# An expert's second quarter of low weight parts, made ahead of the loads of its second half

## The chip, the cores and the metric

The kernel runs on one core of a Trainium2 chip. The metric is the time of one execution on the device in microseconds (us), the median of several runs.

## The reference

The program chains three stages. Its inputs and outputs are fp32.

```python
def _attn_ref(q, k, v, tau):            # 4 x 8 heads, 576 rows, 64 wide
    scores = scale * np.matmul(q, k.transpose(0, 1, 3, 2))
    thresh = np.max(scores, axis=-1, keepdims=True) - tau
    scores = np.where(scores >= thresh, scores, -1000000000.0)
    ...                                 # softmax, then attn @ v

def _moe_ref(x, expert_emb, tau, w1, w2):   # 2304 tokens x 512, 8 experts, F = 1024
    expert_idx = np.argmax(logits, axis=1)
    gate_w = probs[np.arange(N), expert_idx]
    for e in range(E):
        mask = expert_idx == e
        h = np.maximum(x[mask] @ w1[e], 0.0)
        out[mask] = gate_w[mask, None] * (h @ w2[e])

def _moe2_ref(x, w_in, w_out):          # 512 -> 2048 -> 512
    h = x @ w_in
    sp = np.where(h > 20.0, h, np.log1p(np.exp(np.minimum(h, 20.0))))
    return ((h * np.tanh(sp)) @ w_out).astype(np.float32)
```

The change is in the middle stage. With the given inputs the reference sends 213, 375, 233, 231, 281, 362, 418 and 191 tokens to experts 0 to 7.

## The kernel before

**Tokens and slots.** The router sorts the tokens by expert into slots of 128 rows; an expert gets as many slots as its tokens need, rounded up. From the counts above these are 2, 3, 2, 2, 3, 3, 4 and 2 slots, so that experts 0 to 7 begin at slots 0, 2, 5, 7, 9, 12, 15 and 19. The program always runs 25 slots (`SLOTS`); the four left over are worked with the last expert's weights. `start_i` holds the first slot of each expert, `sexp_i` the expert of each slot.

**TensorE** walks the slots in order (`slot(i)` in the TensorE block): `m1` of slot i (x @ w1 in 8 groups), the transposes `t_x` of slot i+1's tokens (L1106), `m2` of slot i-1 (h @ w2), and the transposes `t_h` of slot i's hidden values (L1136). Each product is three fp32r matmuls (`passes`, L1110 to L1112): high part of the data times high part of the weights, high times low, low times high. So for each weight the kernel needs a high part `wh` and a low part `wl`.

**Weights.** An expert has 4 MB of them, handled in 16 chunks of 128x512 (`CH_E`), four chunks to a quarter (`CQ`). Quarters 0 and 1 are w1, quarters 2 and 3 are w2. Each weight is read twice:

- The *high part* comes by a cast load from HBM, fp32 to fp32r, one DMA of 1 MB for each quarter, issued by POOL (`load_quarter`, L605). It goes into one of two halves of `wh`, by the parity of the expert.
- The *raw values* come by DMAs of 256 KB from SP's queue (`chunk`, L475) into `stage`, a ring of four chunks. SP may issue chunk n when POOL has used chunk n-4 (it waits on `w_split`).
- The *low part* is then made by POOL: stage minus wh, one TENSOR_TENSOR for each chunk (`low_parts`, L594, called through `low_quarter`), which counts up `w_split`. It waits for the cast load of its quarter and for its chunk in `stage`.

**What TensorE waits for.** `m1` of a slot of expert e waits for `w_split` to reach 16 e + 8 (quarters 0 and 1 of that expert's low parts are made); `m2` waits for 16 e + 12, and from its fifth group on for 16 e + 16.

**POOL's order.** Experts 0 and 1 are mostly handled during attention and routing. From expert 2 on, POOL runs `next_expert(e, par, n)` once for each expert, in program order: for e = 2 and 3 written out, for 4 to 7 in a hardware loop with two experts in its body. Its steps are

1. wait until `m1` of expert e-2 is done (`m1_done`), then issue the cast loads of quarters 0 and 1 of expert e (here called point A);
2. make the low parts of quarter 3 of expert e-1, then of quarter 0 of expert e;
3. wait until `m2` of expert e-2 is done (`m2_done`), then issue the cast loads of quarters 2 and 3 of expert e (point B);
4. make the low parts of quarters 1 and 2 of expert e.

In the first two of these, POOL also issues the gathers of token rows that are not yet in (`gather`, L631): two after point A of expert 2, five behind expert 2's last low part. POOL, SP and the DMA queues keep the order in which the program names them.

Of the kernel before, what the change touches and what calls it, by code (L numbers as in the profile page):

```python
# [82 lines left out]
def build(nc, qT, kT, v, tau, embT, moe_tau, w1, w2, w_in, w_out, out):  # L83
# [446 lines left out]
    def _(g):  # L530
# [52 lines left out]
        def low_parts(use, high, low, first, chunks=range(CH_E)):  # L583


            for c in chunks:
                if c % CQ == 0 and first[c // CQ] is not None:
                    g.wait_ge(*first[c // CQ])
                g.wait_ge(stg_in[c % STAGES], (use + c // STAGES + 1) * 16)
                src, dst = high(c), low(c)  # L590
                raw = stage[:, c % STAGES, :]
                if len(src.shape) == 3:
                    raw = raw.rearrange("p (a b) -> p a b", a=src.shape[1])
                g.tensor_tensor(dst, raw, src.bitcast(F32), ALU.subtract).then_inc(w_split, 1)  # L594

        def load_quarter(e, par, i):
            a = i * CQ * CHUNK
            dst = wh[:, par, a:a + CQ * CHUNK]
            if i < 2:
                src = w1_e[e, :, 2 * i:2 * i + 2, :]  # L600
                dst = dst.rearrange("p (k f) -> p k f", k=KD // 2)
            else:
                src = w2_e[e, :, (i - 2) * CQ:(i - 1) * CQ, :]
                dst = dst.rearrange("p (c n) -> p c n", c=CQ)
            g.dma_start(dst, src).then_inc(w_cast[par][i], 16)  # L605
# [8 lines left out]
        def low_quarter(e, par, n, i):  # L614

            low_parts(CH_E // STAGES * e,
                      lambda c: wh[:, par, c * CHUNK:(c + 1) * CHUNK],
                      lambda c: wl[:, 1 - par, c * CHUNK:(c + 1) * CHUNK],
                      [(w_cast[par][j], 16 * n) for j in range(QUARTERS)], range(i * CQ, (i + 1) * CQ))
# [9 lines left out]
        def gather(s):  # L629
            got = x_first[s] if s < FIRST else x_near if s < NEAR else x_far if s < FAR else x_next if s < AHEAD else x_last  # L630
            g.indirect_dma_start(x_slot(s), None, x_tok, bass.IndirectOffsetOnAxis(inv_i[:, s:s + 1], 0),  # L631
                                 bounds_check=N - 1, oob_is_err=False).then_inc(got, 16)
# [11 lines left out]
        def next_expert(e, par, n):  # L644

            first = g.value_load(start_i[0:1, bass.ds(e - 1, 1)], min_val=1, max_val=SLOTS)
            g.wait_ge(m1_done, g.snap(first * 2))
            g.sem_inc(pool_passed, 1)
            load_quarter(e, par, 0)
            load_quarter(e, par, 1)  # L650
            if isinstance(e, int) and e == 2:
                for s in range(FAR, AHEAD):
                    gather(s)
            low_quarter(e - 1, 1 - par, n - 1 + par, 3)
            low_quarter(e, par, n, 0)
            g.wait_ge(m2_done, first)
            g.sem_inc(pool_passed, 1)
            load_quarter(e, par, 2)
            load_quarter(e, par, 3)
            low_quarter(e, par, n, 1)  # L660
            low_quarter(e, par, n, 2)

        next_expert(2, 0, 2)
        for s in range(AHEAD, SLOTS):
            gather(s)
        next_expert(3, 1, 2)
        with g.Fori(2, E // 2) as b:
            for par in range(2):
                next_expert(b * 2 + par, par, b + 1)
# [950 lines left out]
```

## Time and profile before

| | |
|---|---|
| median of 3 runs | 1066.23 us (1063.78 to 1070.02) |
| profiled execution, its own time | 1065.5 us |
| its span, first to last instruction | 1063.9 us |
| mean granted TensorE clock | 0.987 of full speed |
| TensorE busy, of the span | 1023.2 us, 96% |
| POOL busy, of the span | 587.7 us, 55% |
| busy in low parts of the experts (L594, `wl`) | 162.8 us, 128 chunks |
| idle of POOL before these | 56.0 us, of which 50.1 us until a chunk had landed in `stage` |
| TensorE idle until a low part was made | 3.4 us, once |

A row of a list of groups reads: line, engine, operation, output<-inputs, shapes, count, busy time and mean ns of one, then the idle time of that engine just before them and what ended it. A busy share is an average over stages with different limits, so it does not tell by itself what an engine's work is worth: attention fills the first 300 us, the experts run from about 326 to 656 us, the last stage follows.

### The profile page before, as it was taken

The page shows a single profiled execution, that of the slowest core. Times are in us where ns is not written, and L with a number is a line of the kernel's source. Part 1 is how long each engine was busy: PE and PEld are TensorE (multiplying, and loading weights), DVE is VectorE, ACT ScalarE, POOL GpSimd, SP SyncE. Part 2 cuts the span into 40 slices and gives each one's busy share as a digit, 9 for nine tenths or more (in the row PEclk, how much of TensorE's full clock was granted, in tenths as well). Part 3 has the DMA queues.
Part 4 walks back from the last instruction along what each step waited for, and adds up shares of the span by engine and source line. Part 5 has one row for each costly group of instructions (what it writes and reads, how often), then busy time and mean ns, then how long its engine had stood idle before and what let it go on. Part 6 is the DMA issues. An engine that isn't in the chain of part 4 may idle for free.

```text
span 1063.9 us, 20987 instructions
## 1 busy us (share of the span) xinstructions
PE 1023.2 (96%) x6712; PEld 850.1 (80%) x6712; DVE 625.7 (59%) x1484; ACT 505.5 (48%) x1020; POOL 587.7 (55%) x672
## 2 busy tenths in 40 slices
PE   7999999999966999899999999999999999999996
PEld 5777777777634888788888889999999999999995
DVE  6998989898764222122222226776676676666653
ACT  5777777777653222222222224555545545555442
POOL 3344444444345868677660627776556565565564
PEclk9999999999987999999999999999999999999999
DMA  8165425441065899998871736400000100000000
GB/s 200 40 169 161 120 81 152 127 125 44 12 220 149 247 287 279 293 295 266 291 240 47 264 104 208 119 31 21 27 14 31 31 10 20 30 30 0 9 22 31
DMA packets 97526, 128.87 MB, mean 121 GB/s; under 512 B 34400, under 2 KB 51808, under 8 KB 96928
## 3 DMA queue, kind: packets, MB, share of 16 engines
q1 hardware_dynamic: 72544, 66.54, 21.8%
q0 software_dynamic: 18880, 53.22, 15.8%
q10 hardware_dynamic: 6016, 7.96, 2.1%
q8 instruction: 53, 0.87, 0.3%
q14 instruction: 33, 0.27, 0.1%
HBM read 111.70 MB, written 16.00 MB: 120 GB/s over the span
## 4 chain that ended last, share of the span: by engine, by line
PE 59%; POOL 4%; DMA 4%; issue 2%; DVE 2%; ACT 1%; another core or an unknown queue 0%; POOLq 0%; SPq 0%; ACTq 0%; DVEq 0%
PE ps L1110 18%; PE ps L1111 18%; PE ps L1112 18%; DMA stage<-w 4%; POOL wl L594 3%; PE ps L1136 1%; PE ps L1048 1%; POOL wh L605 1%; PE ps L1185 1%; PE ps L1106 1%; POOL xs_far L631 1%; PE ps L1058 1%; ACT junk L824 1%; PE ps L997 0%
## 5 line engine op out<-in xcount | busy, mean ns | idle before, releaser
L594 POOL TENSOR_TENSOR wl<-stage,wh 128x512 fp32r<-128x512 f32 x128 | 162.8, 1294 | 56.0 <-DMA stage<-w 50.1
L708 POOL TENSOR_TENSOR mg<-mw,mr 128x384 f32<-128x384 f32 x96 | 117.3, 1222 | 73.7 <-DVE mr L1545 73.2
L766 ACT ACTIVATE ex<-sc,rmin 128x576 f32<-128x576 f32 x144 | 111.6, 776 | 78.0 <-DVE sc L1316 78.0
L714 POOL TENSOR_TENSOR gl<-mg,gh 128x384 fp32r<-128x384 f32 x96 | 98.6, 1028 | 79.1 <-ACT gh L902 78.2
L1110 PE MATMUL ps<-yth,winh 128*128 128x384 f32 x384 | 130.9, 341 | 0.0
L1112 PE MATMUL ps<-yth,winl 128*128 128x384 f32 x384 | 129.5, 337 | 0.0
L1111 PE MATMUL ps<-ytl,winh 128*128 128x384 f32 x384 | 128.8, 335 | 0.0
L1326 DVE SCALAR_TENSOR_TENSOR pm<-sc,thr,ex 128x576 f32<-128x576 f32 x144 | 116.7, 812 | 19.2 <-POOL thr L558 15.3
L1316 DVE TENSOR_SCALAR_CACHE_REDUCE sc<-ps,nscale 128x576 f32<-128x576 f32 x144 | 116.9, 813 | 9.8 <-PE ps L957 9.0
L558 POOL TENSOR_SCALAR thr<-rmin,taup 128x1 f32<-128x1 f32 x144 | 75.4, 524 | 76.2 <-DVE sc L1316 74.2
L1111 PE MATMUL ps<-woutl,gh 128*128 128x512 f32 x288 | 113.5, 394 | 0.0
L1110 PE MATMUL ps<-wouth,gh 128*128 128x512 f32 x288 | 113.0, 392 | 0.0
L1112 PE MATMUL ps<-wouth,gl 128*128 128x512 f32 x288 | 111.9, 389 | 0.0
L894 ACT ACTIVATE ml<-mn,two 128x384 f32<-128x384 f32 x96 | 59.3, 617 | 97.7 <-DVE mn L1526 97.7
L1522 DVE TENSOR_SCALAR mm<-ps 128x384 f32<-128x384 f32 x96 | 53.3, 555 | 88.2 <-PE ps L1112 88.1
L1483 DVE TENSOR_TENSOR xtl<-ps,xth 128x512 fp32r<-128x512 f32 x25 | 17.3, 692 | 130.5 <-ACT xth L839 118.7
L1005 PE MATMUL ps<-pt,vb 128*64 128x128 f32 (+1 forms) x1280 | 93.4, 282 | 0.0
L890 ACT ACTIVATE mm<-mm 128x384 f32<-128x384 f32 x96 | 50.3, 524 | 90.0 <-DVE mm L1522 89.8
L1110 PE MATMUL ps<-wh,xth 128*128 x200 | 81.8, 409 | 7.5 <-POOL wl L594 3.4
L957 PE MATMUL ps<-k_t,q_t 64*128 64x288 f32 x512 | 81.7, 439 | 5.9 <-DMA k_t<-kT 5.9
L854 ACT ACTIVATE hth<-ps 128x512 fp32r<-128x512 f32 x50 | 27.2, 596 | 126.4 <-PE ps L1136 121.1
L1005 PEld LDWEIGHTS ps<-pt,vb 128*64 128x64 f32 (+1 forms) x1280 | 67.0, 135 | 21.6 <-issue 21.6
(193 smaller groups left out, 2253.0 us busy)
## 6 DMA issues: line engine op xcount, KB each, us to landing
stage<-w SPq DMA_DIRECT2D x128, 256.0 KB, 4.5
wh<-w POOLq DMA_DIRECT2D x32, 1024.0 KB, 8.1
y_dense<-yo ACTq DMA_DIRECT2D x25, 256.5 KB
q_t<-qT SPq DMA_DIRECT2D x16, 288.0 KB, 3.6
k_t<-kT SPq DMA_DIRECT2D x16, 288.0 KB, 4.1
vb<-v SPq DMA_DIRECT2D x16, 288.0 KB, 4.5
stage<-w_in SPq DMA_DIRECT2D x16, 256.0 KB, 3.4
winh<-w_in POOLq DMA_DIRECT2D x1, 4096.0 KB, 13.8
```

The source lines that it names most:

```text
L558: g.tensor_scalar(thr[:, i % 2, t:t + 1], rmin[:, i % 2, t:t + 1], taup[:, :], None, ALU.add).then_inc(thr_ready, 1)
L594: g.tensor_tensor(dst, raw, src.bitcast(F32), ALU.subtract).then_inc(w_split, 1)
L708: g.tensor_tensor(mg[:, f % 2, :], mw[:, f % 2, :], mr[:, f % 2, :], ALU.mult).then_inc(g_done, 1)
L714: g.tensor_tensor(gl[:, f % 4, :], mg[:, f % 2, :], gh[:, f % 4, :].bitcast(F32), ALU.subtract).then_inc(gl_ready, 1)
L766: act.activation(ex[:, i % 2, t * S:(t + 1) * S], sc[:, i % 2, t * S:(t + 1) * S], ACT.Exp, bias=rmin[:, i % 2, t:t + 1], scale=-1.0).then ...
L957: m = pe.matmul(s_psum(lane)[:, h, :], q_t[st // HEADS][rows, st % HEADS, q0:q0 + P], k_t[rows, st, h * S // 2:(h + 1) * S // 2], start=Tr ...
L1005: m = pe.matmul(ps[to, OT0:OT0 + P], vb[rows, st, k, :], pt[rows, i % 2, k * P:(k + 1) * P], start=c == 0, stop=c == PAIRS)
L1110: pe.matmul(out_, lhs_h, rhs_h, start=start, stop=False)
L1111: pe.matmul(out_, lhs_h, rhs_l, start=False, stop=False)
L1112: return pe.matmul(out_, lhs_l, rhs_h, start=False, stop=stop)
L1316: dve.tensor_scalar(sc[:, i % 2, t * S:(t + 1) * S].rearrange("p (h n) -> p h n", h=2), s_psum(t), nscale[:, :], BIG, ALU.mult, ALU.min, a ...
L1326: dve.scalar_tensor_tensor(pm[:, i % 2, t * S:(t + 1) * S], sc[:, i % 2, t * S:(t + 1) * S], thr[:, i % 2, t:t + 1], ex[:, i % 2, t * S:(t ...
```

## The change

In `next_expert` the call that makes quarter 1 of the low parts moves from behind point B to ahead of the wait for `m2_done` that stands before it.

```diff
@@ def next_expert(e, par, n):
             low_quarter(e - 1, 1 - par, n - 1 + par, 3)
             low_quarter(e, par, n, 0)
+            low_quarter(e, par, n, 1)
             g.wait_ge(m2_done, first)
             g.sem_inc(pool_passed, 1)
             load_quarter(e, par, 2)
             load_quarter(e, par, 3)
-            low_quarter(e, par, n, 1)
             low_quarter(e, par, n, 2)
```

The order of the chunks, their number and their buffers stay. On all engines but POOL the instructions are the same in the same order. On POOL, for experts 2 and 3, the program before has these instructions (x8 under one row are two quarters of low parts; L605 with 128x2x1024 is a cast load of a w1 quarter, with 128x4x512 of a w2 quarter):

```order
L605 DMA wh<-w 128x2x1024 x2
L631 DMA xs_far<-x_tok,inv_i 128x512 x2
L594 TENSOR_TENSOR wl<-stage,wh 128x512 x8
L605 DMA wh<-w 128x4x512 x2
L594 TENSOR_TENSOR wl<-stage,wh 128x512 x8
L631 DMA xs_far<-x_tok,inv_i 128x512 x5
...
L605 DMA wh<-w 128x2x1024 x2
L594 TENSOR_TENSOR wl<-stage,wh 128x512 x8
L605 DMA wh<-w 128x4x512 x2
L594 TENSOR_TENSOR wl<-stage,wh 128x512 x8
```

In the changed program twelve low parts stand between the two pairs of loads, and four between the second pair and the next expert's first. The same place, with the change:

```order
L605 DMA wh<-w 128x2x1024 x2
L631 DMA xs_far<-x_tok,inv_i 128x512 x2
L594 TENSOR_TENSOR wl<-stage,wh 128x512 x12
L605 DMA wh<-w 128x4x512 x2
L594 TENSOR_TENSOR wl<-stage,wh 128x512 x4
L631 DMA xs_far<-x_tok,inv_i 128x512 x5
...
L605 DMA wh<-w 128x2x1024 x2
L594 TENSOR_TENSOR wl<-stage,wh 128x512 x12
L605 DMA wh<-w 128x4x512 x2
L594 TENSOR_TENSOR wl<-stage,wh 128x512 x4
```

The loads of the w2 quarters moved behind one quarter more of low parts; the loads of the w1 quarters kept their place.

In the loop body, which stands for experts 4 to 7, the same quarter moved past the same pair of loads (one of the two copies; ISA rows are waits with a register's value):

```order
 L594 TENSOR_TENSOR wl<-stage,wh 128x512 x4
+L589 ISA
+L594 TENSOR_TENSOR wl<-stage,wh 128x512 x4
 L605 DMA wh<-w 128x4x512 x2
-L589 ISA
-L594 TENSOR_TENSOR wl<-stage,wh 128x512 x4
 L589 ISA
 L594 TENSOR_TENSOR wl<-stage,wh 128x512 x4
```

## Rows read from the trace of the kernel before

**Rows 1.** The page: two engines' busy time, and the group of low parts.
```profile
PE 1023.2 (96%) x6712; PEld 850.1 (80%) x6712; DVE 625.7 (59%) x1484; ACT 505.5 (48%) x1020; POOL 587.7 (55%) x672
L594 POOL TENSOR_TENSOR wl<-stage,wh 128x512 fp32r<-128x512 f32 x128 | 162.8, 1294 | 56.0 <-DMA stage<-w 50.1
```

**Rows 2.** Who TensorE waited for, 380 to 800 us: total, times, longest.
```profile
PE ps L1110 <- POOL wl L594: 3.4, 1, 3.4
```

**Rows 3.** The chain that ended last, 402 to 446 us: start, us, what.
```profile
405.50 1.51 POOL wh L605 x2
407.03 3.80 POOL wl L594 x3
410.85 7.02 DMA stage<-w
...
437.02 1.51 POOL wh L605 x2
438.55 4.96 POOL wl L594 x4
443.70 0.49 PE ps L1110
```

**Rows 4.** POOL in order of time, 361 to 453 us: start, us, what, [idle before].
```profile
361.80 5.05 POOL L594 TENSOR_TENSOR wl<-stage,wh 128x512 fp32r<-128x512 f32 x4 [3.08 <-DMA stage<-w]
366.78 1.59 POOL L605 DMA_DIRECT2D wh<-w  x2
...
376.85 2.68 POOL L594 TENSOR_TENSOR wl<-stage,wh 128x512 fp32r<-128x512 f32 x2 [3.28 <-DMA stage<-w]
379.84 2.55 POOL L594 TENSOR_TENSOR wl<-stage,wh 128x512 fp32r<-128x512 f32 x2 [0.32 <-DMA stage<-w]
...
405.50 1.51 POOL L605 DMA_DIRECT2D wh<-w  x2
...
415.16 5.32 POOL L594 TENSOR_TENSOR wl<-stage,wh 128x512 fp32r<-128x512 f32 x4 [2.56 <-DMA stage<-w]
420.42 1.42 POOL L605 DMA_DIRECT2D wh<-w  x2
...
437.02 1.51 POOL L605 DMA_DIRECT2D wh<-w  x2
438.55 4.95 POOL L594 TENSOR_TENSOR wl<-stage,wh 128x512 fp32r<-128x512 f32 x4
447.37 5.04 POOL L594 TENSOR_TENSOR wl<-stage,wh 128x512 fp32r<-128x512 f32 x4 [3.86 <-DMA stage<-w]
452.33 1.42 POOL L605 DMA_DIRECT2D wh<-w  x2
```

**Rows 5.** TensorE in order of time: slots 7, 9, 10 and 12 begin.
```profile
415.41 0.48 PE L1110 MATMUL ps<-wh,xth 128*128 x1
...
439.29 1.04 PE L1136 MATMUL ps<-ident,hs 128*128 128x128 f32 x8
443.70 0.49 PE L1110 MATMUL ps<-wh,xth 128*128 x1 [3.37 <-POOL wl L594]
...
457.71 0.48 PE L1110 MATMUL ps<-wh,xth 128*128 x1
...
482.38 0.48 PE L1110 MATMUL ps<-wh,xth 128*128 x1
```

**Rows 6.** Stretches of 4 us: engines' busy us (x), PEclk, DMA share, GB/s.
```profile
436.00:440.00 4.00, 4.00 (x23) 3.33 (x22) 0.32 (x2) 0.08 (x1) 3.98 (x5) 1.00 0.75 199
444.00:448.00 4.00, 4.00 (x12) 3.20 (x12) 0.00 (x0) 0.00 (x0) 0.63 (x1) 0.61 1.13 377
```

**Rows 7.** DMA issues of stretches at 437, 532, 432 and 440: last number, us to landing.
```profile
wh<-w POOLq DMA_DIRECT2D x1, 1024.0 KB, 7.2
wh<-w POOLq DMA_DIRECT2D x1, 1024.0 KB, 9.0
stage<-w SPq DMA_DIRECT2D x1, 256.0 KB, 3.6
stage<-w SPq DMA_DIRECT2D x1, 256.0 KB, 7.4
```

**Rows 8.** Same view at 175 us and at 636 us; then POOL in order of time there.
```profile
wh<-w POOLq DMA_DIRECT2D x1, 1024.0 KB, 5.3
wouth<-w_out POOLq DMA_DIRECT2D x1, 1024.0 KB, 5.7
636.44 1.50 POOL L695 DMA_DIRECT2D wouth<-w_out  x2 [11.88 <-PE ps L1112]
642.25 7.95 POOL L594 TENSOR_TENSOR woutl<-stage,wouth 128x512 fp32r<-128x512 f32 x6 [4.31 <-DMA wouth<-w_out]
```

## The prediction

> **What bounds the kernel now.** I read the page first: TensorE is busy for 96% of the span, POOL for 55% [rows 1]. So a change on POOL can only pay where TensorE waits for POOL. The list of TensorE's waits shows one such place behind 380 us: 3.4 us, once, for a low part of the weights [rows 2]. The chain of waits shows what stands ahead of it: until 443.70 it runs along POOL and the loads into `stage`, from there on along TensorE [rows 3]. TensorE in order of time names the place: it ends slot 8 with the transposes that start at 439.29 and last 1.04 us, and starts the next m1 at 443.70 [rows 5]. That is slot 9, the first of expert 4, whose m1 needs quarters 0 and 1 of that expert's low parts; POOL ends quarter 1 at 438.55 + 4.95 = 443.50 [rows 4]. The need arises at 439.29 + 1.04 = 440.33.
>
> The stall has a second cost. Between 444 and 448 the granted clock is 0.61, against 1.00 before it [rows 6], so part of that stretch ran at the lower of the two levels (1.2 GHz) after TensorE had stood idle. Slot 9 lasts 457.71 - 443.70 = 14.01 us, where slots 10 and 11 take (482.38 - 457.71) / 2 = 12.33 each [rows 5]: 1.7 us lost. So whatever brings expert 4's quarter 1 forward wins at most 3.4 + 1.7 = 5.1 us (0.5%), and whatever delays it costs its delay in full, since nothing later gives it back. I count half a per cent, 5.3 us, as what a measurement of this kernel can tell from no change.
>
> **What sets POOL's pace.** Call A the issue of an expert's first two cast loads, B that of the second two. B stands at 366.78, 405.50 and 437.02 for experts 2, 3 and 4, A at 420.42 and 452.33 for experts 4 and 5 [rows 4]: B to A takes 14.9 and 15.3 us, A to B 16.6. Of the low parts POOL is idle 56 us, 50.1 of it for chunks in `stage` [rows 1]. The first low part of quarter 2 starts late behind B: 376.85 - 366.78 = 10.1, 415.16 - 405.50 = 9.7, 447.37 - 437.02 = 10.4 us [rows 4]. These 10 us hold the two issues (1.5), quarter 1 (5.0) and some 3 us of waiting for chunk 8. That chunk was asked for when chunk 4 was used, and lands 7.4 us after its issue, against 3.6 for one issued at 432, when no cast load was under way [rows 7]. The cast load of quarter 2, issued at 437, has landed in 7.2 us by then [rows 7], hidden behind quarter 1.
>
> **The change, part by part.** Nothing is added or removed: the same 16 low parts, 4 cast loads and 16 chunks for each expert. Three things move.
>
> 1. Quarter 1 comes ahead of the two issues of B. It starts 1.5 us earlier against quarter 0's end, whose chunks are unaffected: they are loaded against A's casts as before. Its own chunks were asked for as quarter 0's were used, with no cast under way, at 3.6 us each; four low parts last 4 x 1.3 = 5.2 us [rows 1], so each chunk has 3.9 us. I take 5.2 us and no wait. The gain is 1.5 us, once, in front of each expert's m1.
>
> 2. B comes 5.2 us later. The wait for `m2_done` ahead of it was over at the earlier B of experts 2 to 4 already (POOL's rows show no idle time there [rows 4]), so it costs nothing 5 us later. SP's queue is not held by it.
>
> 3. Quarter 2 now has no cover: POOL issues B's pair and next needs what the first of them brings. The chunks are no longer the limit, since they were asked for during quarter 1. The trace does not show this order with `wh`, so I bound L, the time from B's first issue to quarter 2's first low part. From below: the fastest cast load of all landed in 5.3 us. The nearest row is w_out's at 636: a pair of 1 MB casts, rows of the same shape, POOL idle behind them, the first landed in 5.7, first low part 642.25 - 636.44 = 5.8 us after the issue [rows 8]. There, no chunk was under way; here the last two of quarter 2's are (issued 1.3 and 0 us before B), and at 377 GB/s [rows 6] 256 KB take 0.7 us. So I take L = 6.5. From above: a first-of-pair under load took 7.2, the slowest 9.0 [rows 7].
>
> The Trainium skill has a rule that speaks against this change: "DMA: Bandwidth & Descriptors", Rules for kernel authors, says to issue a DMA early, compute, and wait for it late. Rows 3 to 5 show the order before doing just that, and by this rule the time goes up.
>
> **The sum.** Before, B to quarter 2 took about 10.1; now quarter 0's end to quarter 2 takes 5.2 + L = 11.7. That is lost for every expert, and it adds up, as A and B follow POOL. With quarter 0 of expert 2 ending as before at 366.8:
> - expert 2: quarter 1 ends 372.0, quarter 2 starts 378.5 (376.85 before, +1.65); before, a 0.32 us wait stood in it [rows 4] that early chunks spare: +1.3. The five gathers and A of expert 3 move by that.
> - expert 3: quarter 0 ends 405.5 + 1.3 = 406.8, quarter 1 at 412.0, where slot 7 needs it at 415.41 [rows 5]: no stall. Quarter 2 starts 418.5 (415.16 before): +3.3.
> - expert 4: A 423.7, quarter 0 ends 437.0 + 3.3 = 440.3, quarter 1 at 445.5. Before: 443.5. So the stall grows from 3.4 to 5.4 us: **+2.0 us**.
>
> Behind it, each expert loses some 1.5 us more of POOL's lead. Expert 4's quarter 2 starts at 445.5 + 6.5 = 452.0 and ends at 457.2, A comes at 457.2 (452.33 before, +4.9). Expert 5's quarter 0 ended 15.7 us behind its A before, so now at 472.9, quarter 1 at 478.1; slot 12 needs it at 482.38 + 2.0 = 484.4. Six us are left, and experts 6 and 7, with more slots ahead of them, have more. The clock's loss of 1.7 us I keep. The profiled execution took 1065.5 us, so 1067.5; the median shown is 0.7 above it, so **1068.2**.
>
> **The rivals.**
>
> *Later still.* The pairs of casts now lie unevenly, B to the next A 12 us instead of 15, and meet chunks and stores of results; L becomes 7.2 to 9.0. With 7.2 the same walk gives delays of 2.0 and 4.8 us behind experts 2 and 3; expert 4's quarter 1 ends at 437.0 + 4.8 + 5.2 = 447.0, 3.5 us later than before: 1069.7. With 9.0 they are 3.8, 8.4, and 7.1 at expert 4: 1073.3. It passes 0.5% from L = 8.1 on. For it: two of three rows of loaded casts are near 8. Against it: the load that made those slow, the chunks of quarter 2, now comes first. 0.15.
>
> *Faster, the exposed cast is short.* If L is under 10.1 - 5.2 = 4.9 us, nothing is lost from expert to expert and the 1.5 us of the two issues remain as a gain: the stall is 1.9 us, 1064.7; if the clock then does not fall, 1.7 less, 1063.0. It decides at L = 4.9. Against it: no cast of 1 MB landed in under 5.3 us. 0.12.
>
> The same page (Anatomy of one DMA) gives 2.0 us plus bytes at 436 GB/s, 4.4 us as its estimate for 1 MB. By that L the time would be 1064.1, or 1062.4 with the clock kept. The rows disagree: 5.3 and 5.7.
>
> *Nothing.* L is 5.3 to 5.8 as on a quiet queue: -0.3 to +0.7 us at expert 4, 1066 to 1067. For it: the row at 636. 0.23, and 0.5 is left for my case with L from 5.8 to 7.2, 1066.9 to 1069.7.
>
> **How the numbers follow.** Likeliest 1068.2. The three runs of before lie from 1063.8 to 1070.0, so a median may be off by 1 to 2 us. The low end takes in half of the faster case, 1064.0; the high end most of the slow one, 1072.5. Faster by over 0.5% would be under 1060.9, beyond even the removal of the stall and its clock loss: 0.03. Slower by over 0.5% is over 1071.6, L above 8.1 with or without noise: 0.09. The rest, 0.88.
>
> **What would show it.** Right: on POOL twelve low parts without long waits in the last four; then two issues and an idle of 4 to 5.5 us before quarter 2, ended by the DMA `wh<-w` and no longer by `stage<-w`; A to A of 33 us instead of 31.9; TensorE's wait for `wl` of about 5.4 us at 440, once. Wrong: if that idle is under 3.4 us, or TensorE's wait is shorter than 3.4 or gone (faster case), if first-of-pair casts take over 7.2 us (later case), or if a second wait for `wl` appears at slot 7, 12 or 15, where I count 3 us or more in hand.

## The result, and the profile after

The changed kernel took 1073.02 us (median of 5 runs, 1069.68 to 1073.67) beside 1067.67 us before (5 runs, 1063.78 to 1070.02): ratio 1.0049, 95% interval 1.0029 to 1.0069. It is slower by 0.5%, 5.35 us between the medians, where 2.0 was forecast. Two more comparisons, among the experiments below, gave 1.0029 and 1.0045. The sign and the place were right, the size was not, and the median lies above the range's end of 1072.5. Of the 4.8 us between the forecast 1068.2 and the measured 1073.02, 3.4 are the size of the move; the other 1.4 are the level, for the median of before rose from 1066.23 to 1067.67 with its last two runs.

The profiled execution took 1069.68 us, its span 1068.0 us: 4.1 us more than the span before. It is the fastest of the five; the others took 1072.6 to 1073.7 us and left no trace. The page of the changed kernel, engines and low parts (before: [rows 1]):

```profile
PE 1024.9 (96%) x6712; PEld 851.3 (80%) x6712; DVE 626.5 (59%) x1484; ACT 505.2 (47%) x1020; POOL 585.6 (55%) x672
L594 POOL TENSOR_TENSOR wl<-stage,wh 128x512 fp32r<-128x512 f32 x128 | 161.9, 1292 | 68.5 <-DMA wh<-w 36.7
```

The work is the same: the same number of instructions on each engine, and busy times within 0.4% of those before. POOL's idle time ahead of low parts rose from 56.0 to 68.5 us, and its largest releaser changed: it was a chunk, `stage<-w`, now it is a cast load, `wh<-w`. TensorE's waits behind 380 us, where 3.4 stood [rows 2]:

```profile
PE ps L1110 <- POOL wl L594: 6.7, 1, 6.7
```

POOL in order of time in the changed kernel, experts 2 to 4, with the issues of the cast loads (L605) and the low parts (L594) (before: [rows 4]):

```profile
372.24 1.58 POOL L605 DMA_DIRECT2D wh<-w  x2
378.76 5.06 POOL L594 TENSOR_TENSOR wl<-stage,wh 128x512 fp32r<-128x512 f32 x4 [4.93 <-DMA wh<-w]
...
412.63 1.51 POOL L605 DMA_DIRECT2D wh<-w  x2
419.06 5.04 POOL L594 TENSOR_TENSOR wl<-stage,wh 128x512 fp32r<-128x512 f32 x4 [4.92 <-DMA wh<-w]
424.05 1.42 POOL L605 DMA_DIRECT2D wh<-w  x2
425.49 5.05 POOL L594 TENSOR_TENSOR wl<-stage,wh 128x512 fp32r<-128x512 f32 x4
435.18 8.70 POOL L594 TENSOR_TENSOR wl<-stage,wh 128x512 fp32r<-128x512 f32 x7 [4.65 <-DMA stage<-w]
445.29 1.26 POOL L594 TENSOR_TENSOR wl<-stage,wh 128x512 fp32r<-128x512 f32 x1 [1.41 <-DMA stage<-w]
446.49 1.51 POOL L605 DMA_DIRECT2D wh<-w  x2
```

Quarter 2 starts 378.76 - 372.24 = 6.5 and 419.06 - 412.63 = 6.4 us behind B, each time when the cast load has landed. B itself comes 5.5 and 7.1 us later than before. Quarter 1 of expert 4 ends at 445.29 + 1.26 = 446.55, 3.05 us later than the 443.50 of before, behind a chunk that was late by 1.41 us. TensorE in order of time, slots 9 and 10 (before: [rows 5]):

```profile
439.00 1.04 PE L1136 MATMUL ps<-ident,hs 128*128 128x128 f32 x8
446.74 0.79 PE L1110 MATMUL ps<-wh,xth 128*128 x1 [6.71 <-POOL wl L594]
...
461.66 0.48 PE L1110 MATMUL ps<-wh,xth 128*128 x1
```

Slot 9 lasts 461.66 - 446.74 = 14.92 us, where it lasted 14.01. The granted clock in stretches of 4 us (columns as in [rows 6]; the clock is the third number from the end) tells why:

```profile
444.00:448.00 4.00, 1.26 (x3) 1.14 (x4) 0.00 (x0) 0.00 (x0) 2.71 (x3) 0.50 0.67 178
448.00:452.00 4.00, 4.00 (x10) 3.06 (x10) 0.00 (x0) 0.00 (x0) 0.00 (x1) 0.50 1.06 312
452.00:456.00 4.00, 4.00 (x20) 3.33 (x19) 0.00 (x0) 1.48 (x3) 2.69 (x3) 0.96 0.96 279
```

TensorE idles from 440.0 on, and the clock stands at 0.50 (1.2 GHz) before the slot begins and until about 452, where before it was at full speed when slot 9 started and then fell for some 3 us (a mean of 0.61 over 444 to 448). So the later start (3.04 us) and the longer slot (0.91 us) make 3.95 of the 4.1 us.

### The profile page after: what moved, and what is told of

Read it like the earlier page. It is cut to its first block, busy times and chain, and to the rows that moved or that the text cites. A ratio compares the mean times of both kernels' runs of the same rounds, so it can differ in the third digit from the quotient of the medians.

```text
span 1068.0 us, 20987 instructions
## 1 busy us (share of the span) xinstructions
PE 1024.9 (96%) x6712; PEld 851.3 (80%) x6712; DVE 626.5 (59%) x1484; ACT 505.2 (47%) x1020; POOL 585.6 (55%) x672
## 4 chain that ended last, share of the span: by engine, by line
PE 64%; POOL 3%; issue 2%; DMA 2%; DVE 1%; ACT 1%; POOLq 0%; SPq 0%; ACTq 0%; DVEq 0%
PE ps L1110 20%; PE ps L1111 20%; PE ps L1112 20%; POOL wl L594 2%; PE ps L1136 2%; DMA stage<-w 2%; PE ps L1048 1%; PE ps L1106 1%; PE ps L1185 1%; PE ps L1058 1%; ACT junk L824 1%; POOL xs_far L631 0%; POOL wh L605 0%; PE ps L997 0%; POOLq L1588 0%
## 5 line engine op out<-in xcount | busy, mean ns | idle before, releaser
L594 POOL TENSOR_TENSOR wl<-stage,wh 128x512 fp32r<-128x512 f32 x128 | 161.9, 1292 | 68.5 <-DMA wh<-w 36.7
L846 ACT ACTIVATE hs<-ps 128x512 f32<-128x512 f32 x50 | 29.9, 598 | 116.3 <-PE ps L1112 116.3
```

## The experiments

My theory: the uncovered cast load of quarter 2 costs POOL time in experts 2 and 3, that time adds up until expert 4's m1, and the move itself gains 1.5 us there. All ratios are to the kernel before, on the same chip, with 95% intervals.

### The move for experts 4 to 7 only

In `next_expert`, e is a Python integer for experts 2 and 3, and a loop register for experts 4 to 7. Against the changed kernel:

```diff
+            early = not isinstance(e, int)
             low_quarter(e, par, n, 0)
-            low_quarter(e, par, n, 1)
+            if early:
+                low_quarter(e, par, n, 1)
             g.wait_ge(m2_done, first)
             ...
             load_quarter(e, par, 3)
+            if not early:
+                low_quarter(e, par, n, 1)
```

> The move is made only for experts 4 to 7; experts 2 and 3 keep the order before. My theory: the delay of the changed kernel is lost in experts 2 and 3 (exposed cast loads, +1.3 to +2 us each) and added up until expert 4's m1; the move itself brings expert 4's quarter 1 forward by 1.5 us. So TensorE's wait for wl at 440 falls from 3.4 to 1.9 to 2.6 us, and the time from the kernel before's by 0.8 to 1.5 us, up to 3.2 where the clock stays up (ratio 0.997 to 0.999). A to A of experts 5 to 7 still lengthens by 1.5 to 3 us without a wait of TensorE. Rival, the delay arises at expert 4 itself (its chunks or its loads): the wait is 5 us or more and the time is that of the changed kernel, ratio 1.003 to 1.006.

Measured: 1064.01 us, ratio 0.9976 (0.9959 to 0.9993), 2.3 us under the 1066.34 of before in the same comparison. That is faster than both kernels. TensorE's wait at slot 9 is 2.79 us, and POOL in order of time of this run shows quarter 0 and 1 of expert 4, then B and the exposed cast load behind them:

```profile
432.20 5.05 POOL L594 TENSOR_TENSOR wl<-stage,wh 128x512 fp32r<-128x512 f32 x4 [2.70 <-DMA stage<-w]
437.60 4.97 POOL L594 TENSOR_TENSOR wl<-stage,wh 128x512 fp32r<-128x512 f32 x4 [0.36 <-DMA stage<-w]
442.51 1.51 POOL L605 DMA_DIRECT2D wh<-w  x2
450.37 5.05 POOL L594 TENSOR_TENSOR wl<-stage,wh 128x512 fp32r<-128x512 f32 x4 [6.34 <-DMA wh<-w]
```

B to quarter 2 is 7.9 us here, and it costs nothing, for behind slot 9 TensorE does not wait for `wl` again. The wait is above the 1.9 to 2.6 expected: A of expert 4 stands at 423.02 here, 2.6 us later than in the first trace of before, behind waits of 1.9, 2.0 and 0.7 us for chunks in expert 3. The rival, a delay that arises at expert 4 itself, falls: the move is a gain there.

### The move for experts 2 and 3 only

The same edit, with the other experts chosen:

```diff
-            early = not isinstance(e, int)
+            early = isinstance(e, int)
```

> The move is made only for experts 2 and 3; experts 4 to 7 keep the order before. My theory: point A of expert 4 comes at about 424 us as in the changed kernel, its point B at 440.7, quarter 1 ends 6.5 us later, at 447.2 or more; TensorE's wait for wl is 7 to 8 us, longer than in the changed kernel (6.7), and the time 3.7 to 4.5 us plus some 1 us of clock over the kernel before, ratio 1.004 to 1.006. Rival, the delay arises at expert 4 itself: wait 3.4 us, ratio 1.000.

Measured: 1071.57 us, ratio 1.0052 (1.0036 to 1.0068), 5.2 us over before in the same comparison. The list of its waits:

```profile
PE ps L1114 <- POOL wl L594: 9.1, 1, 9.1
```

The wait is above the 7 to 8 us expected: L of expert 3 was 8.0 us, where the changed kernel's first trace has 6.4 (B at 413.19, quarter 2 at 421.22). The loss is made in experts 2 and 3 alone. The two halves of the move, +5.2 and -2.3 us, add up to 2.9 us, a little under the 3.2 to 5.35 us that the three comparisons of the whole change give.

### The pair of loads split

```diff
             g.wait_ge(m2_done, first)
             g.sem_inc(pool_passed, 1)
             load_quarter(e, par, 2)
+            low_quarter(e, par, n, 1)
             load_quarter(e, par, 3)
-            low_quarter(e, par, n, 1)
             low_quarter(e, par, n, 2)
```

> Point B is split: cast load of quarter 2, low parts of quarter 1, cast load of quarter 3, low parts of quarter 2. My theory: the loss of the change is the cast load of quarter 2 without cover; here quarter 1 covers it (5.2 us of 5.7) and the chunks of quarter 2 meet one cast load instead of two, so quarter 2 starts about 7 to 8 us behind B instead of 9.7 to 10.4. Expert 2 and 3 then gain some 2 us each, expert 4's quarter 1 ends before 441 and TensorE's wait is 0 to 1 us: time 3 to 5 us under the kernel before, ratio 0.995 to 0.997. Rival, the loads as a whole (8 MB an expert) set the pace of POOL: whatever quarter 2 wins the next quarters lose by later loads, A to A stays at 31 to 32 us, ratio 0.999 to 1.001.

Measured: 1061.67 us, ratio 0.9960 (0.9942 to 0.9978). One of the 12 executions took 3516.9 us, for a reason that no trace shows; the others lie between 1059.9 and 1066.9. POOL in order of time of this run, expert 3:

```profile
403.97 0.77 POOL L605 DMA_DIRECT2D wh<-w  x1
404.76 3.82 POOL L594 TENSOR_TENSOR wl<-stage,wh 128x512 fp32r<-128x512 f32 x3
409.18 1.28 POOL L594 TENSOR_TENSOR wl<-stage,wh 128x512 fp32r<-128x512 f32 x1 [0.61 <-DMA stage<-w]
410.41 0.77 POOL L605 DMA_DIRECT2D wh<-w  x1
411.99 5.04 POOL L594 TENSOR_TENSOR wl<-stage,wh 128x512 fp32r<-128x512 f32 x4 [0.81 <-DMA stage<-w]
416.98 1.43 POOL L605 DMA_DIRECT2D wh<-w  x2
```

Quarter 2 starts 411.99 - 403.97 = 8.0 us behind B, released by a chunk. At experts 2 and 4 it is 9.3 and 9.1 us, above the 7 to 8 expected. Expert 4's quarter 1 ends at 440.1, and no wait of TensorE for `wl` is left in the trace. A repeat on another chip:

> The split pair once more, on the chip of the changed kernel's third measurement: ratio 0.994 to 0.998, no wait of TensorE for wl or one under 1.5 us.

Measured: 1062.09 us, ratio 0.9971 (0.9954 to 0.9987), again without a wait for `wl`; quarter 1 of expert 4 ends at 438.5. Quarter 2 of expert 3, though, starts 9.6 us behind B:

```profile
403.48 0.77 POOL L605 DMA_DIRECT2D wh<-w  x1
...
413.11 5.03 POOL L594 TENSOR_TENSOR wl<-stage,wh 128x512 fp32r<-128x512 f32 x4 [2.69 <-DMA stage<-w]
```

At experts 2 and 4 it is 9.4 and 10.1 us, hardly better than the 9.6 to 10.9 of before. The rival, that all loads together set the pace, falls by the time: both intervals end below its 0.999. A to A is 29.2 and 29.7 us in the first of these traces and 30.5 and 30.9 us in the second, where the rival had 31 to 32. That the gain is made between B and quarter 2, as I expected, is not shown. What the two traces share is that POOL ends expert 4's quarter 1 earlier than in any trace of before (443.1 at the earliest), so that the wait is gone.

### The two loads of point B exchanged, in both kernels

```diff
-            load_quarter(e, par, 2)
             load_quarter(e, par, 3)
+            load_quarter(e, par, 2)
```

In the changed kernel:

> The changed kernel with the two loads of point B in the other order, quarter 3's first: quarter 2's cast load lands as the second of its pair, which adds 1.8 us to the exposed time (5.7 against 0.75 + 6.7 us at 636 in the trace of before). My theory (the exposed cast load is the price, once for each of experts 2 and 3): L is 8.3 us, expert 4's quarter 1 ends 3.6 us later than in the changed kernel, TensorE's wait is 10 to 11 us and the time 3 to 4 us over the changed kernel's, ratio 1.007 to 1.009. Rival, POOL's pace is set by all loads together: what quarter 2 loses the later quarters win back, and the time stays within 1 us of the changed kernel's.

Measured: 1077.18 us, ratio 1.0097 (1.0077 to 1.0118), 7.5 us over the changed kernel's 1069.69 in the same comparison, twice what was expected. L is 382.25 - 372.18 = 10.1 and 428.62 - 416.96 = 11.7 us, so the two experts lost 3.6 and 5.2 us more instead of 1.8 each. At expert 3:

```profile
416.96 1.51 POOL L605 DMA_DIRECT2D wh<-w  x2
428.62 5.04 POOL L594 TENSOR_TENSOR wl<-stage,wh 128x512 fp32r<-128x512 f32 x4 [10.15 <-DMA wh<-w]
```

Together that is 8.8 us, and quarter 1 of expert 4 ends 9.0 us later than in the changed kernel's first trace. So the exposed load is paid for once by each expert, as I held, but the price that I gave it was wrong. TensorE's waits for `wl` are 14.0 us in all, 7.3 more than in that trace: 10.4 at slot 9, 2.3 at slot 7 and 1.3 in the m2 of slot 8, for the last quarter of expert 3.

In the kernel before:

> The kernel before with the two loads of point B in the other order. My theory: there quarter 1 and the wait for a chunk cover a cast load of up to 10.1 us; as the second of its pair quarter 2's lands 0.75 + 9.4 = 10.15 us behind B, so the same edit that costs the changed kernel 3 to 4 us costs 0 to 1 us here, ratio 0.999 to 1.002, and the wait of quarter 2 is now ended by the cast load. Rival, the cover has no such slack: 3 us, ratio 1.003.

Measured: 1074.29 us, ratio 1.0068 (1.0044 to 1.0091): a clear miss. I had read the second cast's landing as 9.4 us from a row that counts two issues, and its last number is the median over both: with 7.2 for the first, the second took 11.6. The landings in this run, at 411.5 and at 412.5 us:

```profile
wh<-w POOLq DMA_DIRECT2D x1, 1024.0 KB, 7.8
wh<-w POOLq DMA_DIRECT2D x1, 1024.0 KB, 12.8
```

The second of a pair lands at 0.75 + 12.8 = 13.6 us here, beyond the 10 us of cover, and quarter 2 starts 13.7 us behind B (411.71 to 425.38). So the cover of the kernel before was worth 10 us and had none to spare. Even with the loads in their own order it was used up once, in the third trace of before, at expert 3:

```profile
415.21 3.79 POOL L594 TENSOR_TENSOR wl<-stage,wh 128x512 fp32r<-128x512 f32 x3 [1.93 <-DMA wh<-w]
```

### TensorE kept busy through the wait

```diff
         def slot(i):
+            if i == 9:
+                for _ in range(50):
+                    pe.transpose(ps[:, INV0:INV0 + P], ident[:, :], ident[:, :])
             m1(i, expert_of(i))
```

> The changed kernel, with 50 transposes of the identity into an unused bank of PSUM ahead of slot 9's m1 (some 5.5 us of work in the wait of 6.7 us; outputs unchanged). My theory: of the changed kernel's cost 0.9 us (trace: slot 9 takes 14.9 us against 14.0, and 12.33 in the others) is the lower granted clock behind a longer idle stretch. With TensorE kept busy the clock stays at 1.00, slot 9 takes 12.3 to 12.6 us and the time is 2.3 to 2.6 us under the changed kernel's, ratio to the kernel before 1.002 to 1.003. Rival, slot 9's length is not the clock's doing (weights or low parts late within it): it stays at 14.9 us, ratio 1.005.

Measured: 1069.62 us, ratio 1.0035 (1.0015 to 1.0054). TensorE in order of time:

```profile
439.91 5.62 PE L1170 MATMUL ps<-ident 128*128 128x128 f32 x50
445.28 0.48 PE L1110 MATMUL ps<-wh,xth 128*128 x1
...
457.62 0.48 PE L1110 MATMUL ps<-wh,xth 128*128 x1
```

The granted clock stays at 1.00 from 440 to 460, and slot 9 takes 457.62 - 445.28 = 12.34 us, as the others. So the rival falls, and the excess of slot 9 is the clock's doing. As time it does not show: the ratio lies above the 1.002 to 1.003 expected, and its interval overlaps those of the changed kernel. In this execution quarter 1 was ready at 443.9 and the transposes ran on for 1.4 us, which takes back half of what the clock gave.

### Both kernels again: what varies

The two kernels without any edit, profiled again.

> The changed kernel once more, for its spread and a second trace. Open: its trace explains 4.1 us over the kernel before, its median was 5.35 us over it. My theory: POOL's time from A of expert 4 to the end of quarter 0 varies by some 3 us between executions, by when the chunks land, and goes into TensorE's wait in full; this trace shows the same L (6.4 to 6.8 us) and a wait for wl between 5 and 9 us; ratio 1.004 to 1.006. Rival, the cost is larger than the wait and the clock explain: the ratio is 1.005 or more while the wait stays at 6.7 and slot 9 at 14.9 us.

> The kernel before, a second trace, to see what varies from one execution to the next without the change: TensorE's wait for wl between 2 and 5 us, quarter 2 starting 9.5 to 10.5 us behind B for experts 2 and 3, released by a chunk and not by the cast load; time 1063 to 1069 us.

> The changed kernel a third time, since its two measurements so far (1.0049 and 1.0029) differ. My theory, that the wait of slot 9 takes up whatever POOL's chunk waits happen to be: ratio between 1.003 and 1.005, the trace's wait plus the length of slot 9 over 12.33 explains its time over the kernel before's within 1 us. Rival, a cost outside the experts that one measurement had and the other not: a part of the trace outside 340 to 460 us is longer by over 1 us.

> The kernel before, a third trace. By its second trace (wait 8.3 us, execution 1070.7 us) the wait of slot 9 varies far more than the 3.4 us that the prediction took as its value. My theory: execution time minus this wait minus the excess of slot 9 over 12.33 us is constant, 1060.4 us within 0.7 in all traces of before and of the changed kernel. Rival: it is not, and something else varies.

The changed kernel: 1069.69 us, ratio 1.0029 (1.0017 to 1.0042), and 1070.55 us, ratio 1.0045 (1.0031 to 1.0060). The kernel before was run once for each of its two new traces. All six traces, in us (time is that of the traced execution, the excess is slot 9's length over 12.33):

| trace | time | B to quarter 2, experts 2, 3 | quarter 1 of expert 4 ends | slot 9 waits | excess |
|---|---|---|---|---|---|
| before, first | 1065.5 | 10.1, 9.7 | 443.5 | 3.4 | 1.7 |
| before, second | 1070.7 | 10.3, 10.9 | 447.8 | 8.3 | 2.0 |
| before, third | 1063.5 | 9.6, 9.7 | 443.1 | 0.7 | 0.1 |
| changed, first | 1069.7 | 6.5, 6.4 | 446.6 | 6.7 | 2.6 |
| changed, second | 1069.9 | 6.3, 7.2 | 446.1 | 6.2 | 2.8 |
| changed, third | 1072.8 | 6.7, 8.5 | 450.3 | 8.5 | 2.2 |

Several of these expectations missed. The changed kernel's second comparison gave 1.0029 where I expected 1.004 to 1.006, and its L at expert 3 was 7.2, above 6.8. The second trace of before has a wait of 8.3 us where I expected 2 to 5, and took 1070.7 us, above 1069.

The wait of 3.4 us, from which the prediction starts, is one draw among 0.7, 3.4 and 8.3. The second trace of before got its 8.3 us in experts 3 and 4, from late chunks:

```profile
417.86 2.68 POOL L594 TENSOR_TENSOR wl<-stage,wh 128x512 fp32r<-128x512 f32 x2 [4.32 <-DMA stage<-w]
422.22 2.59 POOL L594 TENSOR_TENSOR wl<-stage,wh 128x512 fp32r<-128x512 f32 x2 [1.69 <-DMA stage<-w]
...
446.49 1.26 POOL L594 TENSOR_TENSOR wl<-stage,wh 128x512 fp32r<-128x512 f32 x1 [0.98 <-DMA stage<-w]
```

Quarter 1 of expert 4 ends at 444.8 on average before and at 447.7 in the changed kernel, 2.9 us later; the excess is 1.3 against 2.5. That makes 4.1 us, within what the three comparisons give (3.2 to 5.35 us). With three traces of each kernel, which lie up to 4.7 us apart, this average could as well be 2 us off.

My theory that the rest of the execution is constant held in four of the six traces (time less wait less excess is 1060.4 to 1060.9) and failed in both third ones, with 1062.7 and 1062.1. There TensorE started slot 1 at 341.96 and 341.44, behind an idle stretch of 3.0 us, where the first trace of before had 340.12 and 1.7 us:

```profile
341.96 0.50 PE L1110 MATMUL ps<-wh,xth 128*128 x1 [2.98 <-issue]
```

So something outside POOL's chain varies by up to 2 us, in both kernels. It lies ahead of slot 9: from the start of slot 10 to the end of the span all six traces take 606.2 to 606.9 us (1063.9 - 457.71 and 1068.0 - 461.66 in the first ones), so behind the wait the change costs nothing. What that idle stretch waits for, the profile does not name. The late start also explains the short wait of before's third trace in part, since TensorE came to slot 9 some 2 us later; there POOL itself waited 0.6 us for TensorE, twice. And in the changed kernel's third trace it is the part that wait and excess leave open: these explain 5.6 of the 7.3 us over before's first trace, where I expected them to explain it within 1 us.

## Why the prediction came out as it did

- **What bounds the kernel: right.** One wait, at slot 9, released by quarter 1 of expert 4. The runs that moved this point moved the time, and what happened on POOL behind it did not in the six traces of the two kernels (606.2 to 606.9 us from slot 10 on).
- **The uncovered cast load: right, its size short at expert 3.** L = 6.5 was forecast. The five traces with this order at experts 2 and 3 and the loads as they were (three of the changed kernel, the move for 2 and 3, and TensorE kept busy) have 6.3 to 6.7 at expert 2, but 6.4, 6.5, 7.2, 8.0 and 8.5 at expert 3, 7.3 on average. Why it is longer there is open. The idle time, its releaser and the single wait are as forecast, and the faster rival with L under 4.9 us is out. The formula of the Trainium skill ("DMA: Bandwidth & Descriptors", Anatomy of one DMA) gives an estimate of 4.4 us for 1 MB; no exposed load here was that short. The Trainium skill's rule in the same page's Rules for kernel authors, to issue a DMA early and wait for it late, held: giving the cover away cost 0.3 to 0.5%.
- **Adding up: right.** For quarter 2 of experts 2 and 3, A of expert 4 and the end of its quarter 1 the walk gave 378.5, 418.5, 423.7 and 445.5; the first trace shows 378.76, 419.06, 424.05 and 446.55. From A to A it has 33.7 and 34.3 us where 33 was forecast. The two halves of the move have opposite signs, as the runs with half the experts show.
- **Failed in the first trace: 16.6 us from A to B, and 5.2 us "and no wait" for quarter 1.** From A of expert 4 to the end of its quarter 1 I took 16.6 + 5.2 = 21.8 us. The first trace shows 22.5, and with 0.35 us from ahead of it this is the 1.05 us by which its quarter 1 ends later than forecast. The row behind "no wait" I read wrongly: the chunk that landed in 3.6 us was asked for at 432, and A's second cast load, issued at 421.2, landed only 11.8 us later. In the first trace the fourth chunk of quarter 1 was asked for at about 435.18 + 4 x 1.24 = 440.1 and used at 445.29, 5.1 us later, though both cast loads had landed by 435.7; a store of results (`y_dense`) was under way, whose part was not tested. Yet over several traces the term stands, and the miss of the first is a draw of the spread: the others show 20.8, 22.5 and, with TensorE kept busy, whose POOL program is the changed kernel's, 19.9. Over these four quarter 1 of expert 4 ends at 446.7, some 2 us later than in before's three, as forecast.
- **Failed: "The clock's loss of 1.7 us I keep".** It was 2.6 in the first trace, and on average 2.5 where before has 1.3. Before, TensorE ran the first microsecond of slot 9 at full clock; behind the waits of 6 us and more it begins at 1.2 GHz. With TensorE kept busy through the wait there is none of it. With the term above (1.05) these 0.9 us turn the forecast 2.0 into the 3.95 us of the first pair of traces.
- **Failed: one execution taken as the level.** The sum started from a wait of 3.4 us, and the range took the spread as 1 to 2 us. The wait itself spreads from 0.7 to 8.3 us in before, and executions of the changed kernel vary with it. The first comparison's 5.35 us is on the high side of the three, and 1.4 us above what its two traces explain. Why its medians lie further apart than those of the others is not settled.

The later rival (L from 7.2 on) came true at expert 3 in two of the changed kernel's three traces, not at expert 2. So it is not a case of its own but part of the spread.

## What to carry to other kernels

When work is moved from behind the issue of a load to ahead of it, ask what covers that load now: here 5 us of cover were given away for 1.5 us of earlier work, once for each expert ahead of the one that is waited for. Splitting the pair, with the load that is needed first before the work and the other behind it, beat the kernel before by 0.3 and 0.4% in two comparisons, and with it the changed kernel. Where a single wait sets the time, take several traces before putting a number on it, since it collects the spread of everything ahead of it. And the last number in a row of DMA issues is a median over the issues that the row counts: for two unequal transfers it is neither.

## What was new about the hardware

- The second of two 1 MB cast loads issued together landed 12.8 to 13.3 us after its issue when chunk loads were under way (exchanged loads in the kernel before, experts 2 and 3), the first in 7.8 to 8.8. At expert 3 the order of the two issues alone was worth 4 us (quarter 2 at 13.7 instead of 9.7 us behind B).
- What a stall costs in clock is not proportional to it: waits of 0.7, 2.8, 3.4, 6.2, 6.7, 8.3 and 8.5 us were followed by 0.1, 1.7, 1.7, 2.8, 2.6, 2.0 and 2.2 us of excess in slot 9.
